# The second MLP's down pairs with their operands exchanged: h stationary, weights moving, output rows on the partitions

## The reference

```python
x = sigmoid(x @ w_gate) * (x @ w_val) @ w_out      # first MLP
out = ((x @ w_a) * (x @ w_b)) @ w_out              # second MLP, 2304 x 512
```

## Time and profile before

| what | value |
|---|---|
| median of three runs | 952.65 us (952.37 to 953.88) |
| the profiled execution | 953.6 us, of it 951.8 us span |
| TensorE matmuls busy | 936.0 us, 5988 instructions |
| TensorE weight loads busy | 865.4 us |
| VectorE busy | 625.7 us |
| ScalarE busy | 481.1 us |
| DMA | 222 MB, 234 GB/s over the span |
| share of TensorE in the chain that ended last | 94% |

### The profile page before, as it was taken

The page is one execution under the profiler, slowest core; times in us unless marked ns, Lnnn a source line. Parts: engine busy times, 40 slices in busy tenths (PEclk is TensorE's granted clock), DMA queues, the critical chain, the costliest instruction groups (busy, mean ns, idle before and its releaser), DMA issues.

```text
span 951.8 us, 16436 instructions
## 1 busy us (share of the span) xinstructions
PE 936.0 (98%) x5988; PEld 865.4 (91%) x5988; DVE 625.7 (66%) x1299; ACT 481.1 (51%) x959; POOL 189.4 (20%) x277
## 2 busy tenths in 40 slices
PE   6899999999999999999999999999999999999998
PEld 5899988888888888888899999999999999999998
DVE  6778686566656667546758475857666758554766
ACT  5777775577556756533344335425254434434333
POOL 4143333333134132333432000000010000000000
PEclk9999999999999999999999999999999999999999
DMA  9869879767948846946674386767796676776762
GB/s 222 216 202 294 230 214 317 193 191 213 302 149 247 232 115 213 299 142 232 242 286 133 140 335 243 253 255 266 259 337 223 247 267 252 270 270 243 247 252 99
DMA packets 146448, 222.33 MB, mean 234 GB/s; under 512 B 80832, under 2 KB 100288, under 8 KB 144064
## 3 DMA queue, kind: packets, MB, share of 16 engines
q1 hardware_dynamic: 129408, 170.55, 54.4%
q0 software_dynamic: 15360, 50.34, 16.4%
q10 hardware_dynamic: 1600, 0.39, 0.2%
HBM read 178.78 MB, written 42.47 MB: 232 GB/s over the span
## 4 chain that ended last, share of the span: by engine, by line
PE 94%; DMA 1%; ACT 0%; issue 0%; DVE 0%; DVEq 0%; ACTq 0%
PE ps L624 16%; PE ps L626 15%; PE ps L625 15%; PE ps L751 13%; PE ps L753 13%; PE ps L752 13%; PE ps L616 2%; PE ps L581 2%; PE ps L592 1%; DMA out<-ost 1%; PE ps L567 1%; PE ps L568 1%; PE ps L764 0%; PE ps L787 0%; ACT ost L1014 0%
## 5 line engine op out<-in xcount | busy, mean ns | idle before, releaser
L624 PE MATMUL ps<-x_hi,gv_hi 128*128 128x512 f32 (+1 forms) x480 | 178.5, 372 | 0.4 <-DVE gv_lo L1151 0.4
L626 PE MATMUL ps<-x_hi,gv_lo 128*128 128x512 f32 (+1 forms) x480 | 176.6, 368 | 0.0
L625 PE MATMUL ps<-x_lo,gv_hi 128*128 128x512 f32 (+1 forms) x480 | 176.3, 367 | 0.0
L751 PE MATMUL ps<-xc,wc 128*128 128x384 f32 x504 | 171.3, 340 | 0.0
L753 PE MATMUL ps<-xc,wc 128*128 128x384 f32 x504 | 170.3, 338 | 0.0
L752 PE MATMUL ps<-xc,wc 128*128 128x384 f32 x504 | 170.2, 338 | 0.0
L1264 DVE TENSOR_TENSOR tt<-ps,tt 128x384 f32<-128x384 f32 x108 | 59.3, 556 | 85.5 <-PE ps L753 85.1
L232 POOL DMA_DIRECT2D w_raw<-in_moe_w_gate x60 | 45.6, 759 | 330.3 <-DVE wo_lo L1158 318.9
L624 PEld LDWEIGHTS ps<-x_hi,gv_hi 128*128 128x128 f32 x480 | 90.2, 188 | 12.0 <-issue 1.2
L626 PEld LDWEIGHTS ps<-x_hi,gv_lo 128*128 128x128 f32 x480 | 90.1, 188 | 11.4
L625 PEld LDWEIGHTS ps<-x_lo,gv_hi 128*128 128x128 f32 x480 | 90.2, 188 | 10.9
(11 more groups left out here) (111 smaller groups left out, 1637.9 us busy)
## 6 DMA issues: line engine op xcount, KB each, us to landing
wc<-wprep SPq DMA_DIRECT2D x54, 1024.0 KB, 6.9
wc<-wprep SPq DMA_DIRECT2D x54, 768.0 KB, 5.7
wprep<-p_out SPq DMA_DIRECT2D x18, 1792.0 KB, 7.4
w_raw<-in_moe_w_gate POOLq DMA_DIRECT2D x60, 256.0 KB, 3.6
w_raw<-in_moe_w_val POOLq DMA_DIRECT2D x60, 256.0 KB, 4.2
w_raw<-in_moe_w_out POOLq DMA_DIRECT2D x60, 256.0 KB, 4.3
v_nat<-in_v SPq DMA_DIRECT2D x58, 128.0 KB, 5.7
q_nat<-in_q SPq DMA_DIRECT2D x48, 96.0 KB, 5.0
```

The source lines that it names most:

```text
L624: pe.matmul(dst, w_h, m_h, start=first, stop=False)
L625: pe.matmul(dst, w_h, m_l, start=False, stop=False)
L626: return pe.matmul(dst, w_l, m_h, start=False, stop=last)
L751: pe.matmul(dst, w_h, m_h, start=k in (0, 1, 3) and t == 0, stop=False, skip_group_check=True)
```

## The change

In the down pairs the operands change places. The sums of h, 128 tokens at a time, are stationary; the weight sums move, 256 features at a time, which are two runs of 128 columns, one of each unit's half of the slot. A block of 384 tokens is three token tiles; unit 0 takes tiles 0 and 1 (512 columns of one bank), unit 1 takes tile 2 (256 columns). `acc` becomes 6 token tiles by 512 features, which is the layout of the output. The snapshots and adds keep their number and order, and take 512 and 256 columns where they took 384 and 384. Each product of a down pair has 18 matmuls of 256 columns for both units where it had 12 of 384.

`turn_out`, `copy_out`, `last_turns`, `ost` and `fin` go. GpSimd stores each of the first two supers with one DMA from `acc` once all eight sums of its last down pair are made, and the opening snapshot of the next super waits for that store. The last super is stored in five parts: SyncE stores three blocks of 384 tokens by 256 features as they are made and the first two tiles of the fourth, ScalarE its last tile. The up pairs' products are the same as before; their temporaries in `tt` lie in another order.

```diff
+HALF_DM = DM // 2
+TILES = BW // P
+UNIT_TILES = (range(0, 2), range(2, TILES))
...
-        acc = place("acc", A_ACC, [P, KT, SUPER])
+        acc = place("acc", A_ACC, [P, 2 * TILES, DM])
...
-        fin = place("fin", A_XR, [P, 6, DM])
-        ost = place("ost", A_OST, [P, 2, DM])
...
+        def by_tile(flat):
+            return flat.rearrange("p (i n) -> p i n", n=HALF_DM)
+
+        def unit_columns(u):
+            tiles = UNIT_TILES[u]
+            return slice(tiles[0] * HALF_DM, (tiles[-1] + 1) * HALF_DM)
+
+        def result(g, u, i):
+
+            if kind_of(g)[0] == "up":
+                return full(i)
+            return by_tile(bank(i, 0, len(UNIT_TILES[u]) * HALF_DM))
+
         def ch(g, u):
-            return full(banks2(g, u)[0])
+            return result(g, u, banks2(g, u)[0])
 
         def b5(g, u):
-            return full(banks2(g, u)[1])
+            return result(g, u, banks2(g, u)[1])
 
         def b2(g, u):
-            return full(banks2(g, u)[2])
-
-        def t11(u):
-            return tt[:, 3 * u, :]
-
-        def t22(u):
-            return tt[:, 3 * u + 1, :]
-
-        def t12(u):
-            return tt[:, 3 * u + 2, :]
+            return result(g, u, banks2(g, u)[2])
+
+        def held_at(g, u, i):
+
+            if kind_of(g)[0] == "up":
+                return tt[:, 2 * i + u, :]
+            return by_tile(tt[:, 2 * i:2 * i + 2, :].rearrange("p u n -> p (u n)")[:, unit_columns(u)])
...
         def acc_of(i, j, u):
 
-            return acc[:, u + 2 * i, j * BW:(j + 1) * BW]
+            tiles = UNIT_TILES[u]
+            return acc[:, j * TILES + tiles[0]:j * TILES + tiles[-1] + 1, i * HALF_DM:(i + 1) * HALF_DM]
...
             for s in range(SUPERS - 1):
-                for i in range(6):
-                    n = 6 * s + i
-                    pool.wait_ge(out_copied, n + 1)
-                    pool.dma_start(out[s * SUPER + i * P:s * SUPER + (i + 1) * P, :],
-                                   ost[:, n % 2, :]).then_inc(out_stored[n % 2], 16)
-            for i in range(2):
-                pool.wait_ge(out_stored[i], 16 * 3 * (SUPERS - 1))
+                for made in (c11, c22, c12, c21):
+                    for u in range(2):
+                        pool.wait_ge(made[u], PAIRS2 * (s + 1))
+                pool.dma_start(out[s * SUPER:(s + 1) * SUPER, :].rearrange("(i p) n -> p i n", p=P),
+                               acc[:, :, :]).then_inc(out_stored, 16)
+            pool.wait_ge(out_stored, 16 * (SUPERS - 1))
+
+        def store_last(eng, i, first, last):
+
+            at = (SUPERS - 1) * SUPER
+            eng.dma_start(out[at + first * P:at + last * P, i * HALF_DM:(i + 1) * HALF_DM].rearrange(
+                              "(i p) n -> p i n", p=P),
+                          acc[:, first:last, i * HALF_DM:(i + 1) * HALF_DM]).then_inc(last_stored, 16)
...
-            for i in range(6):
-                sp.wait_ge((fin_act, fin_dve)[i % 2], i // 2 + 1)
-                tile = (3, 4, 5, 0, 1, 2)[i]
-                at = (SUPERS - 1) * SUPER + tile * P
-                sp.dma_start(out[at:at + P, :], fin[:, tile, :]).then_inc(fin_stored, 16)
-            sp.wait_ge(fin_stored, 6 * 16)
+            for made, i, j in ((c11, 0, 0), (c22, 1, 1), (c12, 0, 1)):
+                for u in range(2):
+                    sp.wait_ge(made[u], ALL_PAIRS)
+                store_last(sp, i, j * TILES, (j + 1) * TILES)
+            sp.wait_ge(c21[0], ALL_PAIRS)
+            store_last(sp, 1, 0, 2)
+            sp.wait_ge(last_stored, 5 * 16)
...
             def product(g, k, u):
 
-                dst = (ch, b5, ch, b2, ch, b5, ch)[k](g, u)
+                b = banks2(g, u)[(0, 1, 0, 2, 0, 1, 0)[k]]
                 slot = (2 * g + (k >= FIRST_K[0])) % WC_SLOTS
                 at = (k if k < FIRST_K[0] else k - FIRST_K[0]) * KW
-                for t in range(2):
-                    w_h, w_l = (wc[:, slot, u, i, at + t * P:at + (t + 1) * P] for i in range(2))
-                    m_h, m_l = operands(g, k, t)
-                    pe.matmul(dst, w_h, m_h, start=k in (0, 1, 3) and t == 0, stop=False, skip_group_check=True)
-                    pe.matmul(dst, w_h, m_l, start=False, stop=False, skip_group_check=True)
-                    mm = pe.matmul(dst, w_l, m_h, start=False, stop=t == 1, skip_group_check=True)
+
+                def three(dst, s_h, s_l, m_h, m_l, opens, closes):
+
+                    pe.matmul(dst, s_h, m_h, start=opens, stop=False, skip_group_check=True)
+                    pe.matmul(dst, s_h, m_l, start=False, stop=False, skip_group_check=True)
+                    return pe.matmul(dst, s_l, m_h, start=False, stop=closes, skip_group_check=True)
+
+                opens = k in (0, 1, 3)
+                if kind_of(g)[0] == "up":
+                    x_at = (K * (g // PAIRS2) + k) % XC_SLOTS
+                    for t in range(2):
+                        w_h, w_l = (wc[:, slot, u, i, at + t * P:at + (t + 1) * P] for i in range(2))
+                        m_h, m_l = (xc[:, x_at, i, t * BW:(t + 1) * BW] for i in range(2))
+                        mm = three(full(b), w_h, w_l, m_h, m_l, opens and t == 0, t == 1)
+                else:
+
+                    for tile in UNIT_TILES[u]:
+                        rows = slice(tile * P, (tile + 1) * P)
+                        for t in range(2):
+                            w_h, w_l = (wc[:, slot, :, i, at + t * P:at + (t + 1) * P] for i in range(2))
+                            to = (tile - UNIT_TILES[u][0]) * HALF_DM
+                            mm = three(bank(b, to, to + HALF_DM), hc_hi[:, t, k, rows], hc_lo[:, t, k, rows], w_h, w_l,
+                                       opens and tile == UNIT_TILES[u][0] and t == 0, t == 1)
                 mm.then_inc(prod[u], 1)
-
-            def turn_out(s, i):
-
-                n = 6 * s + i
-                if i == 0:
-                    pe.wait_ge(c21[1], PAIRS2 * (s + 1))
-                if n >= 2:
-                    pe.wait_ge(out_copied, n - 1)
-                for t in range(KT):
-                    mm = pe.transpose(bank(2 + n % 2, t * P, (t + 1) * P), acc[:, t, i * P:(i + 1) * P], ident[:, :])
-                mm.then_inc(out_turned, 1)
 
             def pair(g):
...
                 s, q = g // PAIRS2, g % PAIRS2
                 for k in range(K):
-                    if s > 0 and q == 1 and k < 6:
-                        turn_out(s - 1, k)
                     await_operands(g, k)
                     for u in range(2):
                         await_bank(g, k, u)
                         product(g, k, u)
...
-            def last_turns():
...
...
                 if opening(g):
                     if g >= PAIRS2:
-                        act.wait_ge(out_turned, 6 * (g // PAIRS2))
+                        act.wait_ge(out_stored, 16 * (g // PAIRS2))
                     to = acc_of(0, 0, u)
                 act.copy(to, ch(g, u)).then_inc(snap1[u], 1)
...
-            def copy_out(n):
-
-                act.wait_ge(out_turned, n + 1)
-                if n >= 2:
-                    act.wait_ge(out_stored[n % 2], 16 * (n // 2))
-                act.copy(ost[:, n % 2, :], bank(2 + n % 2)).then_inc(out_copied, 1)
...
-            for i, tile, b in ((0, 3, 2), (2, 5, 0), (4, 1, 6)):
-                act.wait_ge(out_turned, 6 * (SUPERS - 1) + i + 1)
-                act.copy(fin[:, tile, :], bank(b)).then_inc(fin_act, 1)
+            act.wait_ge(c21[1], ALL_PAIRS)
+            store_last(act, 1, 2, TILES)
...
-            for i, tile, b in ((1, 4, 3), (3, 0, 1), (5, 2, 7)):
-                dve.wait_ge(out_turned, 6 * (SUPERS - 1) + i + 1)
-                dve.tensor_copy(fin[:, tile, :], bank(b)).then_inc(fin_dve, 1)
```

More of the change, by code:

```diff
@@ L203, in attention_mlp_program @@
         hc_hi_ready, hc_lo_ready = sem("hc_hi_ready"), sem("hc_lo_ready")
-        out_turned, out_copied = sem("out_turned"), sem("out_copied")
-        out_stored = [sem(f"out_stored{i}") for i in range(2)]
-        fin_act, fin_dve, fin_stored = sem("fin_act"), sem("fin_dve"), sem("fin_stored")
+        out_stored, last_stored = sem("out_stored"), sem("last_stored")
         mlp1 = (moe_w_gate, moe_w_val, moe_w_out)
@@ L280, in full, with t11, t22, t12 @@
             return ps[:, i, 0:BW]
+        def by_tile(flat):
[7 more added lines that the diff above has]
+            return by_tile(bank(i, 0, len(UNIT_TILES[u]) * HALF_DM))
         def ch(g, u):
-            return full(banks2(g, u)[0])
+            return result(g, u, banks2(g, u)[0])
         def b5(g, u):
-            return full(banks2(g, u)[1])
+            return result(g, u, banks2(g, u)[1])
         def b2(g, u):
-            return full(banks2(g, u)[2])
-        def t11(u):
-            return tt[:, 3 * u, :]
-        def t22(u):
-            return tt[:, 3 * u + 1, :]
-        def t12(u):
-            return tt[:, 3 * u + 2, :]
+            return result(g, u, banks2(g, u)[2])
[3 more added lines that the diff above has]
```

(44 more changed lines are left out.)

19 lines of the change are left out of this document (2 added, 17 removed).

## The result

| | before | changed |
|---|---|---|
| median of 4 runs | 952.56 us (952.37 to 953.88) | 948.06 us (947.10 to 949.11) |
| profiled execution, its span | 953.6, 951.8 | 949.1, 947.3 |
| ratio, 95% interval | | 0.995 (0.9937 to 0.9962) |
| TensorE matmuls | 5988 | 6294 |

A forecast was written before the change was run, and what follows sets the result against it. TensorE's own matmul stream was taken to bound the second MLP, plus what follows the last product. Down pairs +5.0, turns -6.5 and end -3.0 gave -4.5 us, 948.2 us median; range 944.5 to 954.0 (8 in 10).

The forecast's parts named there:

- The down pairs (+5.0): Nine down pairs in the second MLP: 1134 matmuls at 120.0 ns replace 756 of 384 columns, adding 5.0 us.
- The bounds: Down pairs: price of a 256-column matmul, lower 110 ns (load alone), upper 127 ns.
- the rival built on it: Down pairs: the weight load sets the pace at 127 ns, +13.0 us, 956.2 us; 11 in 100.
- The fixed part hidden (936.9 us): Down pairs: 110 ns a matmul is the price, -6.3 us instead of +5.0, 936.9 us; 7 in 100.
- The records' length as price (1025 us): Down pairs: each load costs its 188 ns record, +82.2 us, 1025 us; 3 in 100.
- The moving operand in two runs: Down pairs: two runs of 128 columns taken as zero cost; rival 2.7 ns a matmul, 951.3 us, 14 in 100.
- the excess: Up pairs' 2.7 ns a matmul over the down pairs, kept as 3.1 us in the range for the two-run operand.
- ScalarE and VectorE: Down pairs' copies and adds: 688 and about 424 ns, 1.11 us for both as before; costed at nothing, hidden by matmuls.
- The turns (-6.5): Supers 1 and 2: removing 48 transposes, 12 copies, 12 stores and their waits saves 3.85 and 2.63 us, -6.5 us.
- The store: GpSimd's single 1.57 MB store a super: covered, cost nothing; rival that it delays weights or opening copy, 950 to 956 us, 5 in 100.
- The end (-3.0): Behind the last product's stream: 3.9 us in place of 6.89, -3.0 us; bounds 3.6 and 5.
- The sum: Whole kernel: +5.0 - 6.5 - 3.0 = -4.5 us, so 948.2 us as median.

The follow-up runs named there:

- the kernel with 128 columns: Changed kernel with each down matmul of 256 columns made as two of 128, each with its own weight load; 1063.88 us.
- one last store: Changed kernel with the last super stored by one DMA of 1.57 MB once all sums are made, in place of five parts; 951.66 us.

## Why the prediction was right, point by point

**The down pairs (+5.0).** Right to 0.1 us: +4.9. The prediction had 120.0 ns, the trace has 119.8. (A straight line through its 227 and 173 ns gives 119; 120.0 is 173.3 less 128 columns at 2.4 GHz.) The bounds were right in kind too: the floor is 111.5 ns, within the 110 to 127 that I took from one run of transposes, and the columns are above it by 8 ns. The upper bound of 127 was too wary, since it added the lag of the load's start and the length to its columns; the rival built on it had 11 in 100 and was decided by a margin of 8 ns.

**The fixed part hidden (936.9 us).** It fell: the fixed part is there at 256 columns. The rival's case was "hardly any fixed part" between the transposes. That fits them: 128 columns are 109 ns apart and the attention's 96 columns 82, so 27 ns for 32 columns and about 2 ns beside them. But this is 0.85 ns a column, twice that of the earlier trace rows, so the transposes are no measure for these matmuls. The Trainium skill's "TensorE: Matmul & The Clock Gate", section "Back-to-back issue gap", has 2.5 ns beside the columns, 109 ns here. It gives this for an isolated matmul and says that in a stream of loads and matmuls both set the spacing, which the prediction left out; the trace disagrees with the 2.5 ns by 11 ns at 256 columns as at 384.

**The records' length as price (1025 us).** It fell, as the kernel with 128 columns shows most plainly. The Trainium skill's "Perfetto Trace Analysis", section "Identifying the Most-Contended Engine", takes the loads' busy share as a measure of how near TensorE is to its limit, beside its share of peak arithmetic; by the loads' share the second MLP had no room before, and half as many loads again went in at no price beyond the fixed part.

**The moving operand in two runs.** Zero, as taken. That the excess hangs on placement, and comes and goes with 128 bytes, I had not seen. The down pairs' pace hangs on it too: with wc moved it was 118.7 ns, 1.3 us less for the nine pairs.

**ScalarE and VectorE.** Costed at nothing, and nothing waits. An add of 512 columns takes 686 to 692 ns and one of 256 418 to 425, for 688 and 424.

**The turns (-6.5).** Right: 5.2 us of transposes, 1.1 of stall, the rest at the switches. That the load of x in the same stretch seems to be the stall's second condition, the prediction did not have.

**The store.** Right that it is covered, and a second one wasn't quite. The sum behind it was off: the store's own pair moved 322 GB/s and not 371, since 3.19 MB of other traffic fell in it and not 4.04; the full pair, at 387, is the one behind it.

**The end (-3.0).** Here the size was off: it is -3.9 us. The step that failed is "from there to the end of the span 2.9 us". I took it from the last of six stores of 256 KB that SyncE issued one behind the other; the 128 KB that ScalarE issues landed after 2.0 us, and from issue to end it is 2.4. The 0.3 us for sharing the DMA engines were not needed either. The time from the stream's end to the end of the last add was taken as 0.62 and is 0.62 us.

**The sum.** By its own steps the change is worth -5.5 us and not -4.5. The profiled executions differ by 4.5, as the clock of the first 35 us cost the changed one 1.0 us more; the medians differ by 4.5, as three of its four executions had a mean clock under 1.00 and only the fourth, at 947.10, had 1.000. That the predicted 948.2 lies 0.1 us from the median is therefore luck: the 0.9 us that the end was under-estimated were largely made up by the clock. The down pairs, the turns and the direction are not luck.

## What to carry to other kernels

To exchange the operands of a matmul, count matmuls and not columns: each costs its columns and a fixed part that two widths in the trace give, as long as that is above the floor that narrower matmuls show (here 111.5 ns, not the 188 of a load's record). Taking away a transposing tail paid here only with the store behind it cut in parts that are issued as they are made; with one store, the end was as long as before. And differences of 1 or 2 us between two executions are compared by stage, since the clock early in a run can hide or feign them. A tile's placement is a size to try by itself where a group of equal matmuls runs slower than its sister.

## What the hardware showed beyond that

- Matmuls of the same shape and type ran 173.3 or 176.0 ns apart depending on where two tiles lay: xc at 16512 bytes with wc at 96512, 176.0; either moved by 128 bytes, 173.3 to 173.8; xc moved by 64, first 173.3 and from the third up pair on 176.7. In the down pairs 119.8 ns fell to 118.7 when wc was moved. The cause is open.
- In the first 35 us the clock made executions of the same work differ: full clock reached only at about 18 us cost 1.1 to 1.3 us (before, and two others), one drop to 1.2 GHz for 3.4 us cost 0.9 us (one last store), two such drops 2.1 to 2.3 us (changed, and before with xc moved).
- Six copies that waited for their stores cost nothing at one super and 1.1 us at another, where a load of 1.57 MB fell in the same stretch and the stores landed after 6.0 us in place of 4.4.
